# Attention inside a feed-forward layer: three short visits of TensorE per slot joined into one, and the steps behind them put in another order

## What is computed

```python
def _attn_ref(q, k, v):                       # q, k, v: (4, 8, 576, 64), factor = 4
    out_d = sm_attn(q_d, k_d, v_d)            # softmax attention over means of 4 positions (144)
    out_up = np.repeat(out_d, factor, axis=2) # the pooled result, each row four times
    mask = np.abs(pos[:, None] - pos[None, :]) < factor
    ...                                       # band attention: each position sees itself and 3 on each side
    return (out_up + out_local).astype(np.float32)

def reference(**kwargs):
    attn_out = _attn_ref(**attn_kwargs)
    x = ...attn_out...reshape(B * S, H * D)   # (2304, 512)
    x = _moe_ref(x=x, **moe_kwargs)           # g = h * sigmoid(h), h = x @ w_in (512 x 2048); g @ w_out
    return _moe2_ref(x=x, **moe2_kwargs)      # g = s * relu(h)**2 + b; g @ w_out
```

## Time and profile before

| | us |
|---|---|
| median of 3 | 968.49 |
| the profiled execution | 968.88 |
| its span (first to last instruction) | 967.1 |
| TensorE busy | 942.9 (97% of the span) |
| GpSimd, VectorE, ScalarE busy | 458.9, 438.4, 363.3 |

### The profile page before, as it was taken

The page is one execution under the profiler, slowest core; times in us unless marked ns, Lnnn a source line. Parts: engine busy times, 40 slices in busy tenths (PEclk is TensorE's granted clock), DMA queues, the critical chain, the costliest instruction groups (busy, mean ns, idle before and its releaser), DMA issues.

```text
span 967.1 us, 15804 instructions
## 1 busy us (share of the span) xinstructions
PE 942.9 (97%) x6071; PEld 868.0 (90%) x6071; DVE 438.4 (45%) x957; ACT 363.3 (38%) x951; POOL 458.9 (47%) x444
## 2 busy tenths in 40 slices
PE   9999999689899999999999999999999999999998
PEld 8899999689899999999999988888888888888897
DVE  5577444745737557366363653233223322422332
ACT  5666343243433434434334652233223222422332
POOL 6677466757759669577483222222221322222222
PEclk9999999989999999999999999999999999999999
DMA  6646453153162433442304532002001000100000
GB/s 164 192 143 179 81 136 82 43 119 89 42 144 47 99 92 81 85 102 49 76 1 139 166 115 66 1 1 87 1 1 65 22 0 0 66 0 0 10 35 22
DMA packets 87169, 68.74 MB, mean 71 GB/s; under 512 B 38720, under 2 KB 73024, under 8 KB 87104
## 3 DMA queue, kind: packets, MB, share of 16 engines
q1 hardware_dynamic: 87104, 67.86, 26.4%
HBM read 52.76 MB, written 15.08 MB: 70 GB/s over the span
## 4 chain that ended last, share of the span: by engine, by line
PE 82%; POOL 7%; issue 5%; DVE 4%; ACT 1%; DMA 0%; SPq 0%; POOLq 0%; ACTq 0%; DVEq 0%
PE pH L801 20%; PE pY L816 20%; PE pH L744 16%; PE pY L749 14%; PE pS L588 3%; POOL weighted L1495 2%; PE pO L636 2%; POOL g_hl L316 1%; POOL x_hl L316 1%; PE pS L591 1%; PE pO L642 1%; POOL vd_f L1449 1%; PE pY L762 1%; PE pO L615 1%; DVE act L1159 1%
## 5 line engine op out<-in xcount | busy, mean ns | idle before, releaser
L316 POOL TENSOR_TENSOR g_hl<-act,g_hl 128x288 fp32r<-128x288 f32 (+2 forms) x208 | 201.6, 970 | 458.4 <-ACT g_hl L840 458.0
L744 PE MATMUL pH<-x_hl,w_in_hl 128*128 128x288 f32 x1518 | 245.4, 303 | 4.9 <-POOL x_hl L316 2.9
L749 PE MATMUL pY<-g_hl,w_out_hl 128*128 128x288 f32 x1536 | 246.2, 300 | 3.5 <-POOL g_hl L316 3.5
L744 PEld LDWEIGHTS pH<-x_hl,w_in_hl 128*128 128x128 f32 x1518 | 213.7, 190 | 9.1 <-issue 5.1
L749 PEld LDWEIGHTS pY<-g_hl,w_out_hl 128*128 128x128 f32 x1536 | 213.9, 189 | 4.7 <-POOL g_hl L316 4.7
L801 PE MATMUL pH<-x_hl,w_in_hl 128*128 128x512 f32 (+1 forms) x960 | 208.4, 368 | 0.0
L816 PE MATMUL pY<-w_out_hl,g_hl 128*128 128x512 f32 x864 | 207.8, 390 | 0.0
L801 PEld LDWEIGHTS pH<-x_hl,w_in_hl 128*128 128x128 f32 x960 | 169.0, 188 | 31.0
L816 PEld LDWEIGHTS pY<-w_out_hl,g_hl 128*128 128x128 f32 x864 | 161.2, 188 | 33.1 <-POOL g_hl L316 0.3
L840 ACT ACTIVATE g_hl<-act 128x288 fp32r<-128x288 f32 (+2 forms) x208 | 104.0, 500 | 207.9 <-DVE act L1159 104.1
L1382 DVE TENSOR_TENSOR act<-act 128x512 f32<-128x512 f32 (+1 forms) x80 | 55.5, 694 | 270.6 <-ACT act L1063 270.6
(11 more groups left out here) (140 smaller groups left out, 773.4 us busy)
## 6 DMA issues: line engine op xcount, KB each, us to landing
qk_f<-qk SPq DMA_DIRECT2D x32, 292.0 KB, 3.6
...
```

Source lines behind the costliest of these rows:

```text
L316: eng.tensor_tensor(lo, full, hi.bitcast(F32), ALU.subtract).then_inc(signal, 1)
L744: last = pe.matmul(pH[:, f % 2, 0:T1], w_in[:, wp, c, f * P:(f + 1) * P], x1[:, par, mp, c, :], start=c + n == 0, stop=c == C - 1 and n == 2)
L749: last = pe.matmul(pY[:, c, 0:T1], w_out[:, wp, f, c * P:(c + 1) * P], g_hl[:, f % RING, mp, 0:T1], start=f + n == 0, stop=f == NF - 1 and ...
```

## The change

1. `ONE_UNIT` becomes one number, 15 (24 in the last slot, 20 in tile 1's, 7 and 31 for two units). There one visit does the pooled sums of the unit two back, the transposes of the unit before, and the scores of this unit, in this order. The pooled sums get columns of `pO` of their own (`pooled`).
2. The copy of the transposes moves from VectorE to ScalarE, where `pooled` does it together with the copy of the sums, after `g_high` of the slot's first up block (in two-unit slots ahead of it) and ahead of `exps`.
3. The band's softmax comes a slot earlier (`SOFTMAX` 1; 4 and 2 in tiles 1 and 2), with `row_shift` and `row_exps` ahead of the second tanh and gate of the slot and `row_normalise` at the start of the next one. GpSimd now starts that slot with two products.
4. The turns move: (4, 24) to (4, 36), (6, 24) to (6, 36), (7, 6) to (7, 2). The tables of sums shift; tile 2 now has four sums in slot 6 (5, 6, 7, 8) where it had three.
5. In the last slot GpSimd does `v_sums` and the first `x_low` ahead of `g_low` of block 15, where all four `x_low` came behind both.

```diff
-SOFTMAX, SOFTMAX_IN = 2, {1: 5, 2: 3}
+SOFTMAX, SOFTMAX_IN = 1, {1: 4, 2: 2}
...
-SUM_IN = {1: {5: (0, 1), 6: (2, 3, 4, 5), 7: (6, 7, 8)}, 2: {3: (0,), 4: (1, 2), 5: (3, 4, 5), 6: (6, 7, 8)}}
+SUM_IN = {1: {5: (0, 1, 2), 6: (3, 4, 5), 7: (6, 7, 8)}, 2: {3: (0,), 4: (1, 2), 5: (3, 4), 6: (5, 6, 7, 8)}}
...
-TURNS = {(4, 24): 0, (6, 24): 1, (7, 6): 2}
-TURNS_IN = {1: {(6, 24): 0, (7, 6): 1, (7, 47): 2}, 2: {(5, 24): 0, (6, 24): 1, (7, 6): 2}}
-
-ONE_UNIT, LAST_UNIT, FIRST_LAST_UNIT = (9, 15, 38), (18, 22, 40), (18, 22, 36)
-TWO_UNITS = (4, 7, 20), (28, 31, 44)
+TURNS = {(4, 36): 0, (6, 36): 1, (7, 2): 2}
+TURNS_IN = {1: {(6, 36): 0, (7, 2): 1, (7, 47): 2}, 2: {(5, 36): 0, (6, 36): 1, (7, 2): 2}}
+
+ONE_UNIT, LAST_UNIT, FIRST_LAST_UNIT, TWO_UNITS = 15, 24, 20, (7, 31)
...
@@ small_rows (TensorE)
+                        if w := unit(h, v - 2):
+                            bank_placed(t, u, k)
+                            if w[0] > NEW:
+                                pe.wait_ge(o_copied, w[0] - H)
+                            attend_unit(w)
+                        if w := unit(h, v - 1):
+                            if not unit(h, v - 2):
+                                bank_placed(t, u, k)
+                            trans_unit(w)
+                        score_unit(unit(h, v))
...
@@ slot_rows (ScalarE)
+                def pooled(h, v):
+                    if w := unit(h, v - 1):
+                        pT_copy(w)
+                    if w := unit(h, v - 2):
+                        evacuate(w)
...
                     g_high(L[0], t, f, 2, T1)
-                    if u == softmax_in(t):
-                        row_exps(t, h)
...
-                    if two:
-                        evacuate(unit(h, now[0] - 1))
-                    elif w := unit(h, now[0]):
-                        exps(w)
+                    if not two:
+                        pooled(h, now[0])
+                        if w := unit(h, now[0]):
+                            exps(w)
                     if u < H - 1:
                         for g in here:
                             place(t, h, g)
+                    if u == softmax_in(t):
+                        row_exps(t, h)
                     for f in more:
                         tanh1(t, f)
...
@@ slot_rows (VectorE)
-                    at_once = 0 if u == softmax_in(t) else 1
-                    for i in sums[:at_once]:
-                        sum_row(t, i)
+                    if u == softmax_in(t) + 1:
+                        row_normalise(t, h)
+                        sums = (None, *sums)
+                    for i in sums[:1]:
+                        if i is not None:
+                            sum_row(t, i)
...
-                    if w := unit(h, now[0] - 1):
-                        pT_copy(w)
...
@@ slot_rows (GpSimd)
+                    finish = u == H - 1 and not late(t, u)
+                    if finish and (w := unit(h, now[0])):
+                        v_sums(w)
+                    if finish:
+                        x_low(t, h, 0)
                     g_low(L[0], t, UPS[u][0], T1)
```

More of the change, by code:

```diff
@@ L200, in __init__ @@
                 self.outs, self.o_down = outs, o_down
+                self.pooled = lambda new: outs[:, HALF + 2 * DQ * new:HALF + DQ + 2 * DQ * new]
                 self.prob, self.prob_d, self.pT, self.pdT = prob, prob_d, pT, pdT
@@ L635, in attend @@
                     elif k < 2:
-                        last = pe.matmul(o.outs[:, HALF:HALF + DQ], vd_s[:, buf, k].rearrange("p h d -> p (h d)"),
+                        last = pe.matmul(o.pooled(by_rows(n)), vd_s[:, buf, k].rearrange("p h d -> p (h d)"),
                                          o.pdT[:, k, :], start=k == 0, stop=k == 1, skip_group_check=True)
@@ L875, in evacuate @@
                     if by_rows(n):
[L876 removed]
+                        copy(o_up(par, u // 2)[mine, :], o.pooled(True)[mine, :]).then_inc(o_copied, 1)
                         return
@@ L975, in slot_rows @@
                     two = len(now) == 2
-                    if (w := unit(h, now[0] - 2)) and not (u == 0 and late(t - 1, H - 1)):
-                        evacuate(w)
+                    finish = u == H - 1 and not late(t, u)
                     if u == 1:
@@ L1006, in slot_rows @@
                     if two:
+                        pooled(h, now[1])
                         exps(unit(h, now[1]))
@@ L1308, in slot_rows @@
                         normalise(w)
+                    if u == softmax_in(t):
+                        row_shift(t, h)
                     if two:
-                        pT_copy(unit(h, now[0]))
                         maxima(unit(h, now[1]))
@@ L1315, in slot_rows @@
                         normalise(unit(h, now[1]))
-                    for i in sums[at_once:]:
+                    for i in sums[1:]:
                         sum_row(t, i)
-                    if u == softmax_in(t) - 1:
-                        row_shift(t, h)
                     if late(t, u):
@@ L1509, in slot_rows @@
                         qk_sums(unit(h, now[1]))
-                    softmax = u == softmax_in(t)
-                    for i in weigh_in(t, u)[:0 if softmax else 2]:
+                    for i in weigh_in(t, u)[:2]:
                         weigh(t, i)
+                    finish = u == H - 1 and not late(t, u)
+                    if finish and (w := unit(h, now[0])):
+                        v_sums(w)
+                    if finish:
+                        x_low(t, h, 0)
                     g_low(L[0], t, UPS[u][0], T1)
@@ L1515, in slot_rows @@
                         qk_sums(w)
-                    if not two and (w := unit(h, now[0])):
+                    if not two and not finish and (w := unit(h, now[0])):
                         v_sums(w)
-                    if u == H - 1 and not late(t, u):
-                        for c in range(C):
+                    if finish:
+                        for c in range(1, C):
                             x_low(t, h, c)
-                    for i in weigh_in(t, u)[:1 if softmax else 0]:
+                    for i in weigh_in(t, u)[2:]:
                         weigh(t, i)
@@ L1526, in slot_rows @@
                         v_sums(unit(h, now[1]))
-                    for i in weigh_in(t, u)[1 if softmax else 2:]:
-                        weigh(t, i)
                     if late(t, u):
```

54 lines of the change are left out of this document (18 added, 36 removed).

## The result

The changed kernel takes 978.22 us (median of 9 runs, 974.29 to 981.71), the kernel before on the same chip 968.27 (966.02 to 970.46): 1.010 times as long, 95% interval 1.0077 to 1.0124. 974.7 was forecast. The profiled execution took 979.32 us, 10.4 more than that of before.

The account below looks back on a forecast made before the run. PE was taken to bound the kernel, busy 942.9 of 967.1 us. Terms -2.7 - 0.6 + 3.8 + 3.8 + 0.3 + 1.2 = +5.8 on 968.9 gave 974.7 us; 8-in-10 range 965.5 to 980.5.

Parts of the forecast that it names:

- the ring: End of tiles: turn 1, placement, tanh, gate, sum, turn 2 form a chain; PE waits 1.8 us at turn 2.
- the late store that makes the keys late: End of tiles 3 and 4: last band stored 2.2 us later, delaying q, k, pooled keys and down 1.
- Visits: Joined visits save part of the fee for returning to large matmuls: 0.07 us each, 38 visits, 2.7 gained.
- Ends of tiles 3 and 4: Late keys, not x, set the start of the next tile: 1.9 us lost each, 3.8 together.
- Of tile 2: End of tile 2: ring and fourth sum in slot 6, wait of 5.3 us, lower clock 1.5; 3.8 lost.
- Of tiles 5 and 6: Ends of tiles 5 and 6: turn 2 and its visit later, partly offset; 0.3 and 1.2 us lost.
- Tile 1: End of tile 1: last two sums end 0.6 us earlier, waits stay and clock falls as before; 0.6 gained.
- the smaller edits: Copies moved to ACT and softmax a slot earlier fit their cover, though copies delay exps by 0.5 us; nothing charged.
- the ring doesn't bind: Rival: ACT's tanh 14 isn't held at the ends of tiles, so turn 2 comes earlier; 966.3 us, 10%.
- tile 1 keeps its clock: Rival: waits in tile 1's slot 7 come apart, and maybe 4.5 us of clock loss return; 970.2 us, 15%.
- the last one: Rival: joined visits are worth their upper bound and the keys land in time; 966.4 us, 9%.
- the clock falls at the new waits: Rival: waits at turn 2 and down 1 in tiles 3 and 4 lower the clock, 1.7 us each; 981.5, 8%.

Follow-up runs that it names:

- j1: The kernel before with the joined visits alone, their copies on ScalarE; 980.72 us, ratio 1.0129 to the kernel before.
- e1: The changed kernel with ScalarE's placement of turns 0 and 1 behind the second tanh of its slot; 973.29 us, ratio 1.0061 to the kernel before.
- e2: The changed kernel with the turns back at their old places; 973.31 us, ratio 1.0062 to the kernel before.
- k1: The changed kernel with v_loc's transfers behind the next tile's first q, k and v, from tile 3 on; 970.96 us, ratio 1.0018 to the kernel before.
- b1: The kernel before with only GpSimd's new order in a tile's last slot; 968.60 us against 968.62, ratio 0.9992.
- e6: The changed kernel with q, k and v loaded ahead of the band's reading and store in two-unit slots; 983.14 us, ratio 1.0153 to the kernel before.
- e4: The changed kernel with sum 5 of tile 2 moved from slot 6 back to slot 5; 977.79 us, ratio 1.0099 to the kernel before.
- e7: The changed kernel with turn 2 at (7,12) and, in the last slot, the visit's VectorE and ScalarE work ahead of x; 972.32 us, ratio 1.0034.

## Why the prediction was right, and where not

The direction, the range and both mechanisms (the ring, and the late store that makes the keys late) held; the total was short by some 4 us. That it came so near is in part luck: tile 1 gained 1.1 us more than I had and the end of tile 2 cost 0.7 less, against losses that I had not priced. By its steps, in the profiled executions (10.4 us apart):

- **Visits** (-2.7 forecast): 0.055 us a slot for 0.07, or 2.1 us over the 38 visits. (The 48 of the forecast are visits; slots of two units have two.) 1.0 us of it stands in slots 2 to 6 of tiles 3 to 5, the rest is inside the numbers of tiles 1 and 2 below. The store of the last band moved by 2.6 where I had 2.2: 1.07 by the joined visit (j1; I had 0.5), 1.1 by the ring (e1), and the remaining 0.4 since x_add is slower (e2 against j1).
- **The ring** (1.8 forecast, 1.56 measured in tiles 3 to 6, 5.05 for 5.3 in tile 2): shown by e1.
- **Ends of tiles 3 and 4** (1.9 each): 1.7, and 3.9, of which 1.6 are the clock behind a wait of 2.26. Keys, not x, set these ends (k1, b1). **Of tile 2**: 3.1 for 3.8. The clock's 1.5 is there: slot 7 takes 14.73, where 9.74 with 5.05 of wait instead of 1.56 would be 13.23, at a clock of 0.88. (Turn 2 there came 1.33 later than before; my own terms, 1.17 + 1.78 - 1.4 - 0.33 + 0.2, give 1.42, not the 1.3 that I wrote.) **Of tiles 5 and 6**: 0.3 and 1.2 for 0.3 and 1.2.
- **Tile 1** (-0.6): -1.7, of it 0.7 in slot 6 and 0.5 in slot 7, with the clock at 0.89 as before and waits of 2.1, 3.4, 2.0 and 2.9 where I had 2.4, 3.5, 2.5 and 3.0. Nearly all of it goes in tile 2, where slots 0 to 5 are 1.4 longer.
- **The failed step** is that one. Under the smaller edits I let the copies delay exps by 0.5 and charged nothing, as normalise is wanted a slot later, and so took the slots of tile 2 up to 5 as ordinary. But its slots 0 and 1 have two units each, and in slot 1 PE waits 1.68 us for the keys of unit 8. POOL's order is v_sums, low part, keys, and v_sums waits for a v that SP issues behind the store of band 5, at 202.50 in both kernels, although the tile began 1.4 us earlier:

```profile
209.81 1.29 POOL L1448 TENSOR_TENSOR vd_f<-vd_f 72x512 f32<-72x512 f32 x1 [2.44 <-DMA vd_f<-vp]
...
212.64 1.14 POOL L1433 TENSOR_TENSOR pair<-qk_f 128x580 f32<-128x580 f32 x1
213.86 0.67 POOL L1437 TENSOR_TENSOR d_f<-pair 128x290 f32<-128x290 f32 x1
```

  The band is copied no earlier than before (202.07 for 202.08), and the rows point at the joined visit. The pooled sums now stand inside up 0 (0.75 us there), so tanh 0 comes 6.0 us behind the start of the tile instead of 5.3, and the copies of transposes and sums now stand between it and exps on ScalarE. After, and the band's copy before:

```profile
200.75 0.41 ACT L882 ACTIVATE act<-pH 128x288 f32<-128x288 f32 x1 [4.17 <-PE pH L739]
201.05 0.28 ACT L835 ACTIVATE pdT<-pO 72x144 f32<-72x144 f32 x1
201.36 0.23 ACT L835 ACTIVATE g_gap<-pO 64x72 f32<-64x72 f32 x1
...
202.07 0.40 ACT L835 ACTIVATE act<-pS 96x306 f32<-96x306 f32 x1
```
```profile
202.08 0.42 ACT L840 ACTIVATE act<-pS 96x306 f32<-96x306 f32 x1
```

  j1, the joined visits alone, has the same wait (1.75) and slot 1 of tile 2 at 11.08 for 9.16; e6, which loads v ahead of the store, takes the wait to 0.28.
- 1.3 us lie where I had no term: 0.3 ahead of tile 1, 0.4 in tile 6, 0.6 in tile 7.
- **Rivals.** That the ring doesn't bind is out (e1), that tile 1 keeps its clock too, and so is the last one: the visits were worth 0.055 and the keys were late. That the clock falls at the new waits came true at one of the seven in tiles 3 to 6 in this execution. It is not a matter of the wait's length alone: over the eight profiles with such waits before down 1 of tiles 3, 4 and 5 (the changed kernel, e1, e2, e4 to e7 and j1) it fell behind 9 of 24, and behind neither of b1's two of 1.5. Waits of 2.10 and 2.03 were followed by a full clock, one of 1.47 (e7, tile 3) by 1.6 us lost. All five of 2.26 and more were followed by a fall. The waits of 1.56 before turn 2 of tiles 3 to 6 were followed by none. I gave this 8% as all or nothing; 9 of 24, times 1.6 us, at three waits is 1.8 us that should have been in the sum.
- **The clock over all runs.** The changed kernel's nine runs have mean granted clocks of 0.982 to 0.991 (the middle one 0.986), the kernel before's fifteen beside e1 have 0.989 to 0.995 (0.993). So a lower clock is part of the 10 us in the unprofiled runs too; my sum had 1.5 us of it, at one place.
